# RWKV attention, feed-forward and gated spatial block: token groups of 2, 3, 3, 2, 2 tiles in place of four of three

## The reference

```python
# attention: 2 x 8 heads, 768 steps, head size 48
for t in range(S):
    cur = einsum('bhd,bhe->bhde', u * kt, vt)
    y[:, :, t] = einsum('bhd,bhde->bhe', rt, state + cur)
    state = wt[:, :, :, None] * state + einsum('bhd,bhe->bhde', kt, vt)
# feed-forward: d_model 384, hidden 1536
xn = (x - mu) / sqrt(var + 1e-6) * g_ln
x = x + maximum(xn @ w_ch1, 0) @ w_ch2
# gated block: d_ff 1024, seq 768
h = maximum(x @ w_in, 0); u, v = h[..., :512], h[..., 512:]
v_n = (v - mean(v)) / sqrt(var(v) + 1e-6)
v_s = einsum('ts,bsd->btd', w_spatial, v_n) + b_spatial[None, :, None]
out = (u * v_s) @ w_out
```

## Time and profile before

| | |
|---|---|
| Median of 3 runs | 429.52 us (428.25 to 430.52) |
| The profiled execution: its time, its span | 431.96 us, 430.2 us |
| Mean granted TensorE clock | 0.968 |
| TensorE (PE) matmul busy | 403.0 us, 94% of the span |
| VectorE (DVE) busy | 224.4 us, 52% |
| ScalarE (ACT) busy | 147.6 us, 34% |
| GpSimd (POOL) busy | 126.4 us, 29% |
| DMA | 24.60 MB, mean 57 GB/s |

### The profile page before, as it was taken

The page is one execution under the profiler, slowest core; times in us unless marked ns, Lnnn a source line. Parts: engine busy times, 40 slices in busy tenths (PEclk is TensorE's granted clock), DMA queues, the critical chain, the costliest instruction groups (busy, mean ns, idle before and its releaser), DMA issues.

```text
span 430.2 us, 12370 instructions
## 1 busy us (share of the span) xinstructions
PE 403.0 (94%) x5260; PEld 374.6 (87%) x5260; DVE 224.4 (52%) x492; ACT 147.6 (34%) x328; POOL 126.4 (29%) x149
## 2 busy tenths in 40 slices
PE   3687879999999999999999899999999999999997
PEld 2676668999999999999999799999988988989897
DVE  3889877666767666657543344133246934312120
ACT  3254544353432323232324422322327722211111
POOL 4656765636452323323220421001015400000000
PEclk9996885899999999999999999999999999999999
DMA  5658541412201020110000200000061100010102
GB/s 165 167 156 247 169 148 49 140 33 66 83 11 53 21 68 3 40 57 2 3 2 3 74 2 0 0 2 2 0 221 35 40 0 0 9 47 21 37 20 91
DMA packets 26555, 24.60 MB, mean 57 GB/s; under 512 B 1666, under 2 KB 23426, under 8 KB 26500
## 3 DMA queue, kind: packets, MB, share of 16 engines
q1 hardware_dynamic: 26500, 23.80, 18.3%
HBM read 21.44 MB, written 2.36 MB: 55 GB/s over the span
## 4 chain that ended last, share of the span: by engine, by line
PE 88%; DVE 5%; issue 3%; POOL 1%; ACT 1%; DMA 1%; SPq 0%; DVEq 0%; POOLq 0%; ACTq 0%
PE odd_bank L1259 11%; PE odd_bank L1261 9%; PE odd_bank L1260 9%; PE low_bank L1178 7%; PE low_bank L1259 6%; PE low_bank L1261 6%; PE low_bank L1260 6%; PE high_bank L1259 4%; PE high_bank L1260 4%; PE high_bank L1261 4%; PE bank L1226 3%; PE bank L1261 3%; PE bank L1260 3%; PE bank L1259 3%; PE bank L1222 2%
## 5 line engine op out<-in xcount | busy, mean ns | idle before, releaser
L611 POOL TENSOR_TENSOR kin<-kin,wtot 128x256 f32<-128x256 f32 x60 | 47.9, 803 | 65.8 <-PE low_bank L1178 59.8
L1178 PEld LDWEIGHTS low_bank<-rin,kin 64*64 64x64 f32 x1728 | 31.3, 144 | 17.7 <-DVE rin L876 7.1
L1178 PE MATMUL low_bank<-rin,kin 64*64 64x32 f32 x1728 | 35.7, 229 | 11.5 <-DMA rin<-in_rT 5.0
L876 DVE TENSOR_TENSOR rin<-rin,wtot 128x256 f32<-128x256 f32 x60 | 36.3, 609 | 14.3 <-PE low_bank L1178 12.2
L1006 DVE SCALAR_TENSOR_TENSOR h10l<-odd_bank,h10h 128x384 fp32r<-128x384 f32 x24 | 13.4, 557 | 44.7 <-ACT h10h L750 44.7
L628 POOL TENSOR_TENSOR vrstd<-vmv,half 128x1 f32<-128x1 f32 x12 | 7.7, 642 | 70.9 <-DVE vmv L1091 70.9
L609 POOL TENSOR_TENSOR kin<-kin,win 128x256 f32<-128x256 f32 x12 | 12.7, 1059 | 49.3 <-PE low_bank L1178 45.7
L918 DVE COPY_PREDICATED near<-msk,low_bank 128x256 f32<-128x256 int32 x54 | 27.0, 552 | 0.0
L1259 PE MATMUL odd_bank<-xnT0h,ffw 128*128 128x384 f32 x66 | 25.0, 379 | 0.0
L750 ACT ACTIVATE h11h<-odd_bank 128x384 fp32r<-128x384 f32 x16 | 7.9, 492 | 47.7 <-PE odd_bank L1261 47.7
L1260 PE MATMUL odd_bank<-xnT0l,ffw 128*128 128x384 f32 x66 | 22.7, 344 | 0.0
(11 more groups left out here) (252 smaller groups left out, 1158.0 us busy)
## 6 DMA issues: line engine op xcount, KB each, us to landing
kin<-in_kT SPq DMA_DIRECT2D x12, 256.0 KB, 3.2
rin<-in_rT SPq DMA_DIRECT2D x12, 256.0 KB, 4.5
win<-in_wT SPq DMA_DIRECT2D x12, 256.0 KB, 3.9
early_stage<-in_w SPq DMA_DIRECT2D x8, 384.0 KB, 4.0
vin<-in_v SPq DMA_DIRECT2D x12, 192.0 KB, 3.0
out<-ob SPq DMA_DIRECT2D x12, 192.0 KB, 1.9
stage<-in_w SPq DMA_DIRECT2D x4, 384.0 KB, 4.3
stage<-in_w_in SPq DMA_DIRECT2D x4, 384.0 KB, 3.3
```

The costliest lines, as they stand in the source:

```text
L611: last = gp.tensor_tensor(k, k, wr[:, :, :, None].to_broadcast([P, NPR, m, c]), ALU.mult)
L876: last = ve.tensor_tensor(r, r, wl[:, :, :, None].to_broadcast([P, NPR, m, c]), ALU.mult)
L1178: mm = te.matmul(dst[s0:s0 + Q, NPR * e + a, :], kin[i % 4][lo:hi, a, s0:s0 + Q], r[:, :, 1, :], start=True, stop=True)
```

## The change

The feed-forward part gets five groups of 2, 3, 3, 2 and 2 tiles (SIZE, FIRST) in place of four of three; first products and U then have 384 or 256 columns. ALONE goes from 4 to 3, so the feed-forward products start at slot 16, and N_BESIDE is 36 of now 60. The order of the w1 and w2 chunks and their slots (LO_SLOTS) move forward to suit, as do the places of the X2T, V and U steps after the scan; tile 10 is turned after the scan and no longer in it. The spatial and output products keep their groups. The diff, cut to its core:

```diff
-ALONE = 4
+ALONE = 3
+    SIZE = [2, 3, 3, 2, 2]
+    NFG = len(SIZE)
+    FIRST = [sum(SIZE[:g]) for g in range(NFG + 1)]
...
-            return b_f1[a] if (step, g) == ("X2T", NG - 1) and a < 2 else b_turn
+            return b_f1[a] if (step, g) == ("X2T", NFG - 1) else b_turn
...
-        FF_PIECES = [(w1, w1s, a) for a in W1_PIECES[:5]] + [(w2, w2s, W2_PIECES[0]), (w1, w1s, W1_PIECES[5])] + \
-                    [(w2, w2s, a) for a in W2_PIECES[1:]]
+        FF_PIECES = [(w1, w1s, a) for a in W1_PIECES[:KC]]
+        for a, b in zip(W2_PIECES, W1_PIECES[KC:]):
+            FF_PIECES += [(w2, w2s, a), (w1, w1s, b)]
+        FF_PIECES += [(w2, w2s, a) for a in W2_PIECES[KC:]]
...
-        LO_SLOTS = [(0, 0), (4, 5), (7, 9), (11, 13), (15, 16), (17, 18), (19, 20), (21, 22), (23, 24),
-                    (25, 26), (27, 28), (29, 30)]
+        LO_SLOTS = [(0, 0), (4, 5), (6, 7)] + [(9 + 2 * n, 10 + 2 * n) for n in range(N_FF - 3)]
...
+        X2T_AT = {0: 2, 1: 9, 2: 14, 3: 19}
+        V_AT = {0: 7, 1: 12, 2: 17, 3: 21}
+        U_AT = {0: 8, 1: 13, 2: 18}
...
-            for n in range(N_BESIDE, NG * NF + 1):
+            for n in range(N_BESIDE, NFG * NF + 1):
...
-                if m == 1:
-                    yield "XT", NG - 1, TG - 1
-                for g, at_x2t, at_v, at_u in ((0, 0, 5, 6), (1, 7, 10, 11), (2, 12, 15, None)):
+                if m in (0, 2):
+                    yield "XT", NFG - 1, m // 2
+                for g in range(NFG - 1):
...
-        TR_STEPS = [("XT", i // TG, i % TG) for i in range(NT - 1)] + [s for s in STEPS if s[0] in ("XT", "X2T")]
+        TR_STEPS = [("XT",) + group_of(i) for i in range(NT - 2)] + [s for s in STEPS if s[0] in ("XT", "X2T")]
...
-                sc.activation(h1[n % 2][0][:, :], f1_bank(n)[:, 0:GT], ACT.Relu).then_inc(h1_hi_ready, 1)
+                t = SIZE[n // NF] * P
+                sc.activation(h1[n % 2][0][:, 0:t], f1_bank(n)[:, 0:t], ACT.Relu).then_inc(h1_hi_ready, 1)
...
-                    split_vn(2 * a)
-                    split_vn(2 * a + 1)
+                    for c in range(CH // 2):
+                        split_vn(CH // 2 * a + c)
...
-                    if n == N_BESIDE:
+                    if n == N_BESIDE + 1:
                         norm(NT - 1)
...
-                for tt in range(TG):
+                for tt in range(SIZE[g]):
                     sl = slice(tt * P, (tt + 1) * P)
                     mm = split_product(b_acc[tt][:, 0:D], h1[n % 2][0][:, sl], h1[n % 2][1][:, sl],
                                        w2s[0][:, w], w2s[1][:, w], f == 0, f == NF - 1)
```

More of the change, by code:

```diff
@@ L59, in rwkv_moe_kernel @@
     GT = TG * P
+    SIZE = [2, 3, 3, 2, 2]
+    NFG = len(SIZE)
+    FIRST = [sum(SIZE[:g]) for g in range(NFG + 1)]
+    assert FIRST[NFG] == NT and max(SIZE) == TG
     W1C, W2C, WIC = KC * F1, NF * D, KC * DFF
@@ L427, in weight_parts, with group_of @@
                         yield n, part
+        def group_of(i):
+            g = max(g for g in range(NFG) if FIRST[g] <= i)
+            return g, i - FIRST[g]
+        X2T_AT = {0: 2, 1: 9, 2: 14, 3: 19}
+        V_AT = {0: 7, 1: 12, 2: 17, 3: 21}
+        U_AT = {0: 8, 1: 13, 2: 18}
         def ff_steps():
-            for n in range(N_BESIDE, NG * NF + 1):
-                if n < NG * NF:
+            for n in range(N_BESIDE, NFG * NF + 1):
+                m = n - N_BESIDE
+                if n < NFG * NF:
                     yield "F1", n // NF, n % NF
@@ L773, in _ @@
             take_x(NT - 1)
-            tr, vu = NT - 1, 0
+            tr, vu = NT - 2, 0
             for step, g, a in STEPS:
@@ L1026, in add_f2 @@
                 dve.wait_ge(f2_done, NF * (g + 1))
-                for tt in range(TG):
-                    i = TG * g + tt
+                for tt in range(SIZE[g]):
+                    i = FIRST[g] + tt
                     ve.tensor_tensor(x[:, i, :], b_acc[tt][:, 0:D], x[:, i, :], ALU.add).then_inc(x2_ready, 1)
@@ L1091, in _ @@
                     ve.tensor_scalar(vmv[:, i, 1:2], vmv[:, i, 1:2], EPS, None, ALU.add).then_inc(v_var_ready, 1)
-                    if g == NG - 1:
-                        split_vn(2 * a)
-                        split_vn(2 * a + 1)
+                    if g == NFG - 1:
+                        for c in range(CH // 2):
+                            split_vn(CH // 2 * a + c)
                     dve.wait_ge(v_rstd_ready, i + 1)
@@ L1100, in _ @@
                     vu += 1
-                if step == "X2" and g == NG - 1:
+                if step == "X2" and g == NFG - 1:
                     weight_lo(N_LATE)
-                elif step == "U" and g == NG - 2:
+                elif step == "U" and g == NFG - 2:
                     weight_lo(N_LATE + 2 + a)
-                elif step == "U" and g == NG - 1 and a < 2:
+                elif step == "U" and g == NFG - 1 and a < 2:
                     weight_lo(N_ALL - 2 + a)
```

95 lines of the change are left out of this document (49 added, 46 removed).

## The result

The changed kernel takes 432.69 us (median of 6 runs, 431.70 to 433.64) where the kernel before took 429.89 us beside it (6 runs, 428.25 to 430.73). The ratio is 1.0069 (95% interval 1.0045 to 1.0094): 0.7% slower, where 429.5 us and no change were forecast. Its profiled execution took 432.51 us, span 430.7, which is close to what the sum gave for that execution (431.86), though its terms miss by 0.5 to 1.3 us each way.

The account below looks back on a forecast made before the run. TensorE was taken as idle or slow before 77.5 us and full after it. Terms -8.7 + 2.1 + 3.2 + 3.3 = -0.1 us on 431.96, less 2.4 to the median, gave 429.5 us; own range 427.4 to 431.7, eight in ten 424.0 to 435.0.

Parts of the forecast that it names:

- The term of -8.7 us: Slots 16 to 27: smaller two-tile products shorten three rounds from 56.7 to 48.0 us if TensorE never waits at full clock.
- the four rivals: Faster, 0.30; slower by low clock in round 4, 0.18; slower by the matmul step, 0.12; slower by VectorE, 0.06.
- Price of the step: A matmul on 256 columns in first products and U: 0.123 us, ends 0.121 and 0.130, at worst 0.174; 432 of them.
- Rival 3: First products and U: weight load bounds the 256-column step at 0.130 us or above, total 432.5, far end 451; chance 0.12.
- Slots 16 to 27: Rounds 4 to 6: -8.7 us from smaller products, +2.1 (0 to +5) for waits, 0.7 a round, tight in the third slot.
- Before slot 16: Earlier weight pieces: ScalarE's cast of chunk 3 holds kt, gain(0) and VectorE, plus GpSimd's extra pieces; +3.2 us (0 to +5).
- chunk 2's hold: Before slot 16: ScalarE held until 25.75 us, delaying attend(0) by 1.5 us, which disappears in the longer hold.
- After the scan: First products +1.6 us, U +0.8, a late w_in chunk +0.9, waits at the last group 0; sum +3.3 (+1 to +5).
- the late chunk of w_in: After the scan: third w_in chunk lands about 8.3 us into the stage, holding ScalarE and a turned xn tile: +0.9 us.
- Rival 2: Round 4: TensorE at 1.2 GHz if the first product comes too late, costing 3.4 us, total 432.8; chance 0.18.

Follow-up runs that it names:

- the second execution: The kernel before, unchanged, profiled once more: that execution took 430.3 us; its runs had a median of 430.55 us, ratio 1.0000.
- the two versions without that wait: Changed kernel with chunk 3's upper half a slot and first x2 transposes a step later, 427.71 us; kernel before with its first x2 transposes two steps later, 427.07 us.
- the new groups alone: Changed kernel with ALONE = 4, so feed-forward products begin in slot 20 as before and steps after the scan come four later: 441.32 us, ratio 1.0255.

## Why the prediction was wrong

**The step that failed** is the first sentence on the sum: it was made "on the profiled execution's 431.96 us", and "the median of the runs is 2.4 below that execution, so I forecast 429.5". That takes the 2.4 us for something that both kernels have. But that execution has 6.8 us of low clock more than the usual 0.976 stands for, at the end of round 4 and in round 5, just where the change works. The term of -8.7 us was the full-clock length of slots 16 to 27 after the change, 48.0, less 56.7. Two further executions have 53.48 and 53.45, and slot 16 at 59.02 and 60.31. So the typical term is -5.5.

By the medians the change gains about 1 us up to the end of the scan (+2.8 in all, +3.7 of it behind), where the sum had 3.4. The sum with the second execution in its place is -5.5 + 2.1 + 3.2 + 3.3 = +3.1 us on 430.3, which is 433.4, and 433.0 on a median of 429.9; measured were 432.69 and 432.52. That this comes within half a microsecond is partly luck: against the second execution slots 16 to 27 gain 2.1 us (the sum has 3.4), slot 16 comes 1.1 later (the sum has 3.2), slots 28 to the last near level gain 0.5 (0) and the rest loses 3.7 (3.3). None of the four rivals asked whether the execution read was typical.

The prediction's reading of the clock, 1.00 up to 63.80 us, is also wrong: the same trace has it at 0.50 from 36.5 to 43.4 and from 50.2 to 57.0 us, so slots before 16 hold low time as well.

**Price of the step**, 0.123: measured 0.119 to 0.120, worth -1.3 to -1.7 us over 432 matmuls. Rival 3 is out. Slots 28 to the scan's end, left as they are in the prediction, lose 0.8 us: 0.5 is the second product of two tiles in slot 28, 0.3 tile 10's turn, which the prediction left out of its sum on both sides of the scan's end.

**Slots 16 to 27**: 50.1 us forecast, 51.36 measured. TensorE's own work was mis-sized: it is busy for 49.27 us where the sum had 48.0. The scan's own 7.0 us a round came from round 6; the same subtraction on round 5 of the old kernel at full clock (19.16 less four first and three second products) gives 7.5. The waits were to be 2.1 us, and TensorE's idle time in the three rounds is 51.36 less 49.27, 2.1. Their place is another than the one named: the view of waits has 0.9 us for xnT's lower half at the end of a round and 0.6 for near, both VectorE's, and none for h1's lower half of the third slot. That TensorE's work does not set the rounds is shown: cutting 3.57 us out of it gave 0.27. GpSimd's pieces are 0.35 us of rounds 4 and 5. What sets the rest is open: each single relief gave from -0.2 to +0.5 us a round, since other waits took its place, and no run relieved all at once.

**Before slot 16**: +3.2 forecast. In the profile +2.67 (1.13 against the second execution); undoing the holds gave 2.1 to 2.7 us. Right in sum, a little high. The mechanism is right in part: ScalarE holds kt as described, but TensorE waits for it 0.4 to 2.9 us and not 3.9, and chunk 2's hold, which was to disappear in the longer one, still keeps own_term and attend(0) waiting for 1.2 us.

**After the scan**: +3.3 forecast, +4.05 measured from the scan's end, by other parts; tile 10's turn is 0.3 of it. The wait for the transpose grew by 0.26, which is what the late chunk of w_in came to in place of 0.9, and was followed by the low clock, 1.5 to 1.6 us, that the sum did not have. The rest can be read by holding the two versions without that wait against each other (118.87 and 116.35 us): TensorE is busy for 117.69 us in place of 115.64, and idle for 1.18 in place of 0.71. Of the 2.05 us of work the steps are 1.0 (24 x 9 x 0.119 less 16 x 9 x 0.174, and 108 steps of U less 72), where the sum had 2.4. The rest is not tile 10's turn, which lies inside both stretches; from start to start it falls on the second products (0.55, the same matmuls), the first (0.3) and U (0.3), as more products follow one another. The idle time is 0.5 for h1's and 0.4 for uT's upper half and 0.3 for x at group ends, for one wait of 0.7 before; I had put these at 0. Rival 2 saw a low stretch, but in round 4, where the clock stayed at 1.00; it fell at the other end of the scan.

## What to carry to other kernels

Before a stretch of the profile enters a sum, look at whether its clock is what the clock usually is there: an execution 2 us above its median has those 2 us somewhere, and if that is where the change works they are not there to be gained. Set the sum against a second execution where one can be had. A wait that nobody minds, such as 2 us of TensorE for a transpose, is worth looking at for itself: moving the first x2 transposes two steps back in the list was worth 2.5 us in the old kernel, where the whole regrouping lost 2.8. And a long wait in the rows is not yet a limit: in rounds 4 to 6 a wait of 3.4 us could be cut to 0.45 and the round was 0.4 us shorter.

## What the runs showed of the hardware

- The clock's low stretches in the first 75 us fall differently in each execution of the same program, and with them slot 16 starts between 57.5 and 60.3 us in three profiles of the old one, and between 58.1 and 63.4 in profiles of the changed one and its variants. The rounds that run at full clock repeat to 0.07 us.
- In the first 30 us and more the views print a clock of 1.00 where the matmuls are as slow as at 0.50: four transposes take 1.12 us at 31.05 us in the changed kernel (printed clock 1.00) and 0.66 at 29.82 in the old one. Three transposes at a printed 0.50 take 0.90 (38.26 us, old kernel), at full clock later 0.49. So the mean clocks of whole executions (0.968, 0.976) leave such time out.
- A wait of 2.2 us of TensorE in the middle of full work was followed by 3.4 us at 1.2 GHz in the changed kernel, in both its profiles, and in four of five of its variants (waits of 2.05 to 2.23 us). The wait of 1.97 us at the same place was not, in two profiles of the old kernel and in that of the new groups alone. Between the transposes at 237.91 us and the fall at 241.79 TensorE was busy for 1.65 of 3.88 us.
- A VectorE instruction that begins beside one of GpSimd's 128x384 pieces ended 0.2 us (xn) or 0.6 us (the decays) after the piece in two kernels: xn of round 5 takes 0.47 us with the piece cut short, 0.76 and 1.02 beside a whole one; the product of decays 0.74, 1.03 and 1.30.
